# Last stage of a three-stage kernel: the low term of the 64-row tail as two 64-row products, issued one behind the other

## The reference

```
rms = np.sqrt(np.mean(x * x, axis=-1, keepdims=True) + 1e-06)
xn = x / rms * rms_g
g = xn @ w_gate                    # [3072, 320] @ [320, 1536]
silu = g * (1.0 / (1.0 + np.exp(-g)))
val = xn @ w_val                   # [3072, 320] @ [320, 1536]
return (silu * val @ w_out)        # [3072, 1536] @ [1536, 320]
```

## Time and profile before

| | us |
|---|---|
| three runs | 883.01, 885.36, 892.77 |
| median | 885.36 |
| profiled execution | 885.66 |
| its span | 883.9 |
| TensorE busy in the span | 825.1 |
| VectorE busy | 512.2 |
| ScalarE busy | 388.0 |

### The profile page before, as it was taken

The page is one execution under the profiler, slowest core; times in us unless marked ns, Lnnn a source line. Parts: engine busy times, 40 slices in busy tenths (PEclk is TensorE's granted clock), DMA queues, the critical chain, the costliest instruction groups (busy, mean ns, idle before and its releaser), DMA issues.

```text
span 883.9 us, 17960 instructions
## 1 busy us (share of the span) xinstructions
PE 825.1 (93%) x6231; PEld 733.6 (83%) x6231; DVE 512.2 (58%) x1055; ACT 388.0 (44%) x694; POOL 135.2 (15%) x190
## 2 busy tenths in 40 slices
PE   6999998259999999999958999999999999999997
PEld 3878776149999999999956888888888888888886
DVE  5588867547787877878824354354453453453332
ACT  5554553047767767677722323323323223222221
POOL 3658776400000000000011001001001001000000
PEclk8999999569999999999987999999999999999999
DMA  6677773599889989899911001001001001000000
GB/s 183 158 197 213 215 206 99 179 295 267 263 269 254 293 247 303 237 285 297 291 45 31 1 1 60 1 1 60 0 0 59 0 0 53 6 0 30 1 1 30
DMA packets 84906, 113.36 MB, mean 128 GB/s; under 512 B 11880, under 2 KB 63624, under 8 KB 84856
## 3 DMA queue, kind: packets, MB, share of 16 engines
q1 hardware_dynamic: 80376, 102.22, 40.0%
q0 software_dynamic: 2304, 7.88, 2.8%
q10 hardware_dynamic: 2176, 2.62, 0.9%
HBM read 96.31 MB, written 16.38 MB: 127 GB/s over the span
## 4 chain that ended last, share of the span: by engine, by line
PE 86%; DMA 4%; issue 3%; DVE 2%; POOL 2%; ACT 2%; SPq 1%; ACTq 1%; DVEq 0%; POOLq 0%
PE psum L1413 45%; PE psum L1488 5%; PE psum L1489 5%; PE psum L1490 5%; PE psum L1437 4%; PE psum L1439 4%; PE psum L1438 4%; PE psum L1281 2%; PE psum L1326 2%; PE psum L1349 2%; PE psum L1302 2%; PE psum L1296 1%; PE psum L1340 1%; PE psum L1405 1%; PE psum L1469 1%
## 5 line engine op out<-in xcount | busy, mean ns | idle before, releaser
L1243 DVE TENSOR_TENSOR gated_lo<-gated,gated_hi 128x512 fp32r<-128x512 f32 x72 | 49.8, 692 | 185.1 <-ACT gated_hi L809 185.1
L804 ACT ACTIVATE sigm_sb<-psum 128x512 f32<-128x512 f32 x72 | 43.1, 599 | 257.1 <-PE psum L1413 257.1
L1413 PE MATMUL psum<-nT_hi,w_gv_hi 128*128 128x512 f32 x432 | 125.7, 399 | 2.6 <-DVE nT_lo L1230 2.6
L1413 PE MATMUL psum<-nT_lo,w_gv_hi 128*128 128x512 f32 x432 | 125.1, 398 | 0.0
L641 POOL DMA_INDIRECT c_rows<-y_by_slot,slot_idx x24 | 22.8, 950 | 553.8 <-DMA y_by_slot<-y_tile 283.4
L1413 PEld LDWEIGHTS psum<-nT_lo,w_gv_hi 128*128 128x128 f32 x432 | 81.9, 190 | 20.1
L1413 PEld LDWEIGHTS psum<-nT_hi,w_gv_hi 128*128 128x128 f32 x432 | 79.3, 190 | 17.1 <-DVE nT_lo L1230 2.8
L1413 PE MATMUL psum<-nT_hi,w_gv_lo 128*128 128x512 f32 x288 | 90.8, 397 | 0.0
L1488 PE MATMUL psum<-w_out_hi,gated_hi 128*128 128x320 f32 x288 | 89.8, 312 | 0.0
L1489 PE MATMUL psum<-w_out_lo,gated_hi 128*128 128x320 f32 x288 | 89.1, 309 | 0.0
L1490 PE MATMUL psum<-w_out_hi,gated_lo 128*128 128x320 f32 x288 | 88.9, 309 | 0.0
(11 more groups left out here) (208 smaller groups left out, 1550.8 us busy)
## 6 DMA issues: line engine op xcount, KB each, us to landing
w_raw<-w SPq DMA_DIRECT2D x38, 640.0 KB, 6.6
w_raw<-w SPq DMA_DIRECT2D x38, 512.0 KB, 4.5
w_raw<-w SPq DMA_DIRECT2D x76, 128.0 KB, 4.8
kv_tok<-tok SPq DMA_DIRECT2D x24, 324.0 KB, 6.7
qk_sb<-qk SPq DMA_DIRECT2D x48, 160.0 KB
y_by_slot<-y_tile SPq DMA_DIRECT2D x12, 321.0 KB, 7.0
og_tok<-o_tok SPq DMA_DIRECT2D x24, 160.0 KB, 6.1
x_tile<-x_by_expert SPq DMA_DIRECT2D x12, 320.0 KB, 2.9
```

Of the source, the lines that this page charges most:

```text
L804: nc.scalar.activation(sigm_sb[f % 2][:], bank[2 * (f % 2)][:], ACT.Sigmoid).then_inc(sig_ready, 1)
L1243: dve.tensor_tensor(gated_lo[f % 4][:], gated[f % 2][:], gated_hi[f % 4][:].bitcast(F32), ALU.subtract).then_inc(hv_lo, 1)
L1413: m = mm(dst, w, x, start=(n == 0), stop=(n == len(terms) - 1))
```

## The change

For each (`t`, `f`) the third product with the low input, of 128 rows, is taken out of the gate's eight and out of the value's eight. In its place stand two products of 64 rows: for the gate the high tail weights in partitions 0 to 63 with `nT_lo[0:64, 2]`, for the value the high tail weights in partitions 64 to 127 with `nT_lo[64:128, 2]`. They are issued one behind the other, between the gate's seven remaining products and the value's seven. For that the value's tail weights are laid out the other way round (low part in partitions 0 to 63, high part in 64 to 127), which `last_low` does for pieces 6 to 11; its loop over the expert steps 4 to 10 becomes two loops, 4 to 6 and 7 to 10. The wait on `hv_ready` moves from ahead of the value's products to ahead of the gate's 64-row product.

```diff
-            def last_low(n):
+            def last_low(n, lows=slice(64, P)):
...
-                dve.tensor_tensor(w_gv_hi[64:P, 2, c], gv_raw[64:P, 2], w_gv_hi[64:P, 2, c].bitcast(F32), ALU.subtract).then_inc(wlast_lo, 1)
+                dve.tensor_tensor(w_gv_hi[lows, 2, c], gv_raw[lows, 2], w_gv_hi[lows, 2, c].bitcast(F32), ALU.subtract).then_inc(wlast_lo, 1)
...
-            with dve.Fori(4, NFULL - 1) as j:
+            with dve.Fori(4, NPIECE // 2 + 1) as j:
                 e_step(j, piece=j - 1)
-            e_step(NFULL - 1, w_next=TS, piece=NFULL - 2)
-            e_step(NFULL, TS, TS, piece=NFULL - 1)
+            with dve.Fori(NPIECE // 2 + 1, NFULL - 1) as j:
+                e_step(j, piece=j - 1, lows=slice(0, 64))
+            e_step(NFULL - 1, w_next=TS, piece=NFULL - 2, lows=slice(0, 64))
+            e_step(NFULL, TS, TS, piece=NFULL - 1, lows=slice(0, 64))
...
             def gate_value(t, f):
                 n = NF2 * t + f
-                for v in range(2):
-                    c = slice(v * F2 + f * P, v * F2 + (f + 1) * P)
-                    if f >= 2:
-                        pe.wait_ge(silu_ready if v == 0 else hv_ready, n - 1)
-                    passes(bank[2 * (f % 2) + v][:], lambda k: w_gv_hi[:, k, c], lambda k: w_gv_lo[:, k, c],
-                           lambda k: nT_hi[:, k], lambda k: nT_lo[:, k]).then_inc(gv_made, 1)
+                gate_bank, value_bank = bank[2 * (f % 2)][:], bank[2 * (f % 2) + 1][:]
+                gate_c, value_c = (slice(v * F2 + f * P, v * F2 + (f + 1) * P) for v in range(2))
+
+                def whole_rows(c):
+                    return ([(w_gv_hi[:, k, c], nT_hi[:, k]) for k in range(KB)] + [(w_gv_hi[:, k, c], nT_lo[:, k]) for k in range(2)]
+                            + [(w_gv_lo[:, k, c], nT_hi[:, k]) for k in range(2)])
+
+                if f >= 2:
+                    pe.wait_ge(silu_ready, n - 1)
+                for k, (w, x) in enumerate(whole_rows(gate_c)):
+                    mm(gate_bank, w, x, start=(k == 0), stop=False)
+                if f >= 2:
+                    pe.wait_ge(hv_ready, n - 1)
+                mm(gate_bank, w_gv_hi[0:64, 2, gate_c], nT_lo[0:64, 2], start=False, stop=True).then_inc(gv_made, 1)
+                mm(value_bank, w_gv_hi[64:P, 2, value_c], nT_lo[64:P, 2], start=True, stop=False)
+                for k, (w, x) in enumerate(whole_rows(value_c)):
+                    m = mm(value_bank, w, x, start=False, stop=(k == 6))
+                m.then_inc(gv_made, 1)
```

More of the change, by code:

```diff
@@ L1135, in _, with e_step @@
                 w2_low(0, r)
-            def e_step(j, w=TE, w_next=TE, piece=None):
+            def e_step(j, w=TE, w_next=TE, piece=None, lows=slice(64, P)):
                 for half in range(2):
@@ L1146, in e_step @@
                 if piece is not None:
-                    last_low(piece)
+                    last_low(piece, lows)
             e_step(0)
```

## The result

The changed kernel takes 900.35 us in the median of four runs (898.72 to 904.54), the kernel before 885.59 in the runs beside it (883.01 to 892.77): 1.0154 times as long, with a 95% interval of 1.011 to 1.0199. The forecast was 897.4 us.

The account below looks back on a forecast made before the run. TensorE bounds the last stage. Two changes of shape and the later half's start, 0.40 us, less the saved 0.233, over 72 steps add 12.0 to 885.66 us: 897.7 profiled, 897.4 us forecast for the median; range 890 to 905 us.

Parts of the forecast that it names:

- What bounds the kernel: Last stage: TensorE never held up, so each nanosecond in its step counts 72 times; 45% of the chain is these products.
- The saved place, 0.233 us a step: Gate and value products: the 64-row pair runs concurrently, fifteen places instead of sixteen, minus 16.8 us in all.
- the third rival of the prediction: 64-row pair: the halves run one behind the other, nothing saved, both changes paid, 28 us more, 913.5 us; chance 0.08.
- The price of a change, 0.195 us, two of them: Into and out of the 64-row pair: 0.09 us emptying plus 0.105 for weights not loaded ahead, at each change.
- The other edits at nothing: Earlier `hv_ready` wait, later banks, `last_low` in other partitions, second loop head: all hidden or negligible, taken as 0.
- The clock: TensorE in the last stage: less dense work, but no change of the granted 1.00 expected, none in the sum.
- The free change of shape: Rival, at the 64-row pair: changes free or covered, only the saving stands, 868.6 us; chance 0.06.
- The hidden loads: Rival, at each change: the array empties but weight loads are hidden, 3 us less, 882 us; chance 0.06.
- The serial halves: Rival, 64-row pair: two 512-column streams run one behind the other, 28 us more, 913.5 us; chance 0.08.

Follow-up runs that it names:

- e3_same_half: The changed kernel with both 64-row products in partitions 0 to 63, so they can't run side by side, value's tail laid out as before: 913.22 us, ratio 1.0312.
- e4_two_visits: The changed kernel with each 64-row product amid its own seven full ones, four changes of shape a step instead of two, nothing side by side: 940.56 us, ratio 1.061.
- e7_bf16_visit: The changed kernel with its two 64-row products reading the upper halves of their numbers as bf16: 888.94 us, ratio 1.0041.
- e1_full_rows: The changed kernel with its two middle products over all 128 rows instead of 64, all other edits kept: 884.49 us against 885.21, ratio 0.9985.
- e5_shared_visit: The changed kernel with the 64-row products of two steps issued in one row in the even step, wait on `hv_ready` stricter: 900.38 us, ratio 1.0153.
- e2_96_rows: The changed kernel with its two middle products over partitions 0 to 95, value's tail laid out as before the change: 885.16 us against 884.65, ratio 0.9993.

## Why the prediction was right

**What bounds the kernel.** Right. Each change in TensorE's step came out 72-fold, and nothing else moved by more than the runs do: the middle stage, from its first transpose to the first product of the last stage, took 287.4 us before and 288.6 after, with 287.0 to 288.7 in the ten experiments, and the gap before the transposes at the turn of a tile went from 0.21 to 0.24. One reading of the page was too generous: the 45% of the chain by `L1413` holds the middle stage's products too, which go through the same helper. In the changed kernel the lines are apart: 14% for the middle stage, 31% for the gate and value of the last.

**The saved place, 0.233 us a step.** Right: the pair starts 0.01 us apart, and taking that away costs 15.4 us in the last stage, where 16.8 was expected (e3_same_half; 12.9 by the medians). That run is also the third rival of the prediction, built: 913.5 us by its sum, 913.22 measured.

**The price of a change, 0.195 us, two of them.** Right in size and in parts. The distance across the way in is 0.33 (0.32 forecast), the records behind both changes are 0.10 too long (0.10 forecast), and 288 changes cost 0.195 each (e4_two_visits; 0.189 by the tiles). The step came out 0.161 longer where 0.167 was forecast, 11.6 us instead of 12.0. The rows that gave the price were of another stage, other shapes and, but for one, another type; they carried over to full and half height with 512 columns without a correction. The rule of the Trainium skill, TensorEngine Tiling (Array Packing), Key Properties, that a change of mode drains TensorE, holds here with 0.09 us. The other half of the price is the load behind it (e7_bf16_visit).

**The other edits at nothing.** Right: 884.49 against 885.21 with all of them and no change of shape (e1_full_rows).

**The clock.** Right: 1.00 from 490 to 897 us, with nothing streaming for 7% of each step (0.4 of 5.65 us).

**The rivals.** The free change of shape was refuted by each row of the visit. Of its argument one half holds: the two products of distinct halves run side by side. The hidden loads are refuted by e7_bf16_visit, where taking the load away is worth the 0.10. The serial halves are refuted by e3_same_half.

**The number.** 897.4 us stands against a median of 900.35, which is inside the range. The last stage explains 11.6 of the 14.8 us between the medians. For the other 3 us I have no cause in the change: the stages ahead are the same code but for the copied loop, e1_full_rows has that loop as well and is not slower, and single executions of either kernel differ by 6 to 10 us. The traces show where such differences come from. Over the profiled executions of the changed kernel and the ten experiments, which all have that loop, the last stage began between 472.3 and 482.0 us; the kernel before's began at 473.1, the changed one's at 482.0, the latest of all. So the 18.9 us between the two profiled executions are 8.9 of scatter ahead of the last stage and 10.0 in it. For the medians of four runs such a split isn't on record, and the 3 us stay a matter of the runs as far as is known.

## What to carry to other kernels

Products of 64 rows in the two halves of the array do run at once, but the way into that shape and back costs about 0.2 us each in fp32r: 0.09 to empty the array, and the whole load of the next weights, 0.10. So a visit pays only if it saves more than 0.4 us, which takes two streams of 512 columns (2 x 0.233); collect several pairs for one visit, and put something with a cheap load right behind each change. When a visit is shared by several steps, look at what else needs the banks earlier: here a piece of VectorE's work that two steps of lead had covered became the bound.

## What the runs showed of the hardware that I had not expected

After three of five waits of TensorE of 2.1 to 2.3 us in the midst of a full stage came a stretch at the lower of its two clock levels (1.2 instead of 2.4 GHz): 0.83 granted in windows of 10 us around them and 1.00 between (e5_shared_visit). The two other waits, 2.08 and 2.27 us long, were followed by no such stretch, so what decides is open. Where it happens, the waits cost more than their own length.

The bf16 products of 512 columns, which read every other half word, were 0.24 us apart inside the visit, no closer than fp32r ones, though their weights loaded in a record of 0.09 to 0.10 us against 0.18 to 0.19.

A product of 96 rows costs no change of shape (e2_96_rows), within 0.2 us in three tiles: 203.1 against 203.3.
